# Filter network of a long convolution: chunk by chunk instead of four chunks at a time, with its decay moved into two tables

## What is computed

```python
h_mlp  = np.maximum(pos_emb @ w1, 0.0) @ w2          # 12480 x 64 -> 64 -> 128
window = np.exp(-0.01 * pos)[:, None]
h_filt = h_mlp * window
u  = x * v                                            # 12480 x 128
Uf = np.fft.rfft(u, n=L, axis=1)                      # L = 2 * 12480
Hf = np.fft.rfft(h_filt, n=L, axis=0)
y  = np.fft.irfft(Uf * Hf[None, :, :], n=L, axis=1)[:, :S, :]
x1 = x * y
x2 = np.maximum(x1 @ moe_w_in, 0.0) ** 2 @ moe_w_out  # 128 -> 2048 -> 128
h  = x2 @ moe2_w_in
out = (h / (1 + np.exp(-1.702 * h))) @ moe2_w_out
```

## Time and profile before

| | us |
|---|---|
| median of 3 runs (lowest, highest) | 1559.16 (1558.95, 1559.96) |
| the profiled execution's own time | 1559.6 |
| its span, first to last instruction | 1557.8 |
| start of the first transform in it | 62.73 |
| TensorE busy in the span | 1532.8 |
| VectorE, ScalarE, GpSimd busy | 992.7, 943.0, 270.0 |
| mean granted TensorE clock | 0.998 of full speed |

### The profile page before, as it was taken

The page is one execution under the profiler, slowest core; times in us unless marked ns, Lnnn a source line. Parts: engine busy times, 40 slices in busy tenths (PEclk is TensorE's granted clock), DMA queues, the critical chain, the costliest instruction groups (busy, mean ns, idle before and its releaser), DMA issues.

```text
span 1557.8 us, 22645 instructions
## 1 busy us (share of the span) xinstructions
PE 1532.8 (98%) x7860; PEld 1458.2 (94%) x7860; DVE 992.7 (64%) x1315; ACT 943.0 (61%) x1217; POOL 270.0 (17%) x313
## 2 busy tenths in 40 slices
PE   7999999999989999999999999999999999999998
PEld 5898889988779999999999999999999999999997
DVE  4867686676656666666666666666666666666664
ACT  3353003431067777777777777777777777777775
POOL 5706791177710000000000000000000000000000
PEclk9999999999999999999999999999999999999999
DMA  7454720743000000000000000000000000000000
GB/s 179 110 83 126 138 41 26 115 113 105 1 0 1 7 10 5 5 5 5 5 5 5 5 5 5 5 5 5 5 5 5 5 5 6 10 5 5 5 7 11
DMA packets 93769, 46.89 MB, mean 30 GB/s; under 512 B 77705, under 2 KB 89337, under 8 KB 93481
## 3 DMA queue, kind: packets, MB, share of 16 engines
q1 hardware_dynamic: 92670, 45.80, 13.2%
q10 hardware_dynamic: 1067, 0.66, 0.1%
HBM read 40.06 MB, written 6.39 MB: 30 GB/s over the span
## 4 chain that ended last, share of the span: by engine, by line
PE 95%; DVE 3%; ACT 1%; issue 1%; DMA 0%; SPq 0%; ACTq 0%; DVEq 0%
PE ps L965 23%; PE ps L967 23%; PE ps L966 23%; PE ps L685 7%; PE ps L737 7%; PE ps L718 6%; PE ps L746 3%; DVE big L561 1%; PE ps L959 1%; PE ps L659 1%; PE ps L673 1%; PE ps L953 1%; PE ps L664 1%; DVE act_lo L940 0%; ACT act_f L890 0%
## 5 line engine op out<-in xcount | busy, mean ns | idle before, releaser
L940 DVE TENSOR_TENSOR act_lo<-act_f,act_hi 128x832 fp32r<-128x832 f32 x480 | 487.0, 1025 | 129.8 <-ACT act_hi L895 121.6
L965 PE MATMUL ps<-act_hi,w_hi 128*128 128x416 f32 x960 | 344.0, 358 | 1.3 <-DVE act_lo L940 1.3
L965 PE MATMUL ps<-in_hi,w_hi 128*128 128x416 f32 x960 | 337.8, 352 | 5.7 <-DVE in_lo L911 3.9
L967 PE MATMUL ps<-act_hi,w_lo 128*128 128x416 f32 x960 | 338.3, 352 | 0.0
L966 PE MATMUL ps<-in_lo,w_hi 128*128 128x416 f32 x960 | 336.0, 350 | 0.0
L966 PE MATMUL ps<-act_lo,w_hi 128*128 128x416 f32 x960 | 335.5, 349 | 0.0
L967 PE MATMUL ps<-in_hi,w_lo 128*128 128x416 f32 x960 | 334.1, 348 | 0.0
L938 DVE CAST act_hi<-act_f 128x832 fp32r<-128x832 f32 x240 | 148.4, 618 | 288.4 <-ACT act_f L890 288.4
L885 ACT ACTIVATE relu<-ps 128x832 f32<-128x832 f32 x240 | 208.3, 868 | 142.7 <-PE ps L967 138.8
L892 ACT ACTIVATE act_f<-ps 128x832 f32<-128x832 f32 x240 | 207.0, 863 | 117.7 <-PE ps L967 117.6
L890 ACT ACTIVATE act_f<-relu 128x832 f32<-128x832 f32 x240 | 216.0, 900 | 22.2 <-DVE act_lo L940 0.3
(11 more groups left out here) (64 smaller groups left out, 1401.2 us busy)
## 6 DMA issues: line engine op xcount, KB each, us to landing
f_ring<-in_fwd SPq DMA_DIRECT2D x52, 240.0 KB, 2.6
u_buf<-in_x SPq DMA_DIRECT2D x20, 312.0 KB
big<-in_v SPq DMA_DIRECT2D x20, 312.0 KB
filter_then_xy<-in_x SPq DMA_DIRECT2D x8, 780.0 KB
out<-rows SPq DMA_DIRECT2D x30, 208.0 KB
big<-in_pos_emb SPq DMA_DIRECT2D x40, 78.0 KB
u_buf<-in_moe_w_in SPq DMA_DIRECT2D x2, 1024.0 KB, 7.5
t<-in_inv ACTq DMA_DIRECT2D x1, 168.8 KB
```

What stands on the lines that cost most here:

```text
L940: nc.vector.tensor_tensor(lo[:, :, :], f[:, :, :], hi[:, :, :].bitcast(F32), ALU.subtract)\
L965: nc.tensor.matmul(to, w_hi[w][:, cols], hi, start=first, stop=False)
L967: return nc.tensor.matmul(to, w_lo[w][:, cols], hi, start=False, stop=last)
```

## The change

- `window` is gone. Since exp(-0.01(120a + b)) is a product of a factor in a and one in b, the factor in b (positive) becomes the per-partition `scale` of the rectification, which is now three ScalarE instructions of 104 columns per chunk (one per pair of positions), and the factor in a goes into a second version of the first transform's table, used for the filter. `t1` holds both and has its own place in SBUF.
- With no window to multiply, `taps` is gone. ScalarE copies the upper three positions of a chunk to SBUF (`copy_high`, 104x384), and VectorE forms both the sum and the difference from PSUM and that copy; GpSimd's part in the network is gone.
- The loops over rounds are written out chunk by chunk on all engines: TensorE does the transposes of chunk n+2, the first layer of n+1 and the second layer of n.
- All of `pos_emb` has a place in SBUF, so its loads wait for nothing. Ten chunks are loaded ahead of the first piece of u, then five chunks and a piece in turn.
- w1, w2 in block-diagonal form and the scales come as one transfer of 128x444; the other tables are loaded from ScalarE's queue behind chunk 4. VectorE folds pieces 0, 1, 2 behind chunks 9, 14, 19, and pieces 3, 4 at groups 3 and 7 of the first transform.
- Four spare products instead of twelve stand ahead of the first transform.

```diff
-    window = np.exp(np.float32(-0.01) * np.arange(S, dtype=np.float32)).reshape(A, B)[:, order]
+    decay_b = np.exp(-0.01 * b)[order].reshape(NCH * HB, 2).T
+    decay_a = np.exp(-0.01 * B * a)
+    net = np.concatenate([twice(w1), twice(w2), np.repeat(decay_b, FO, axis=0)], axis=1)
+    return {"fwd1": np.concatenate([fwd1, fwd1 * decay_a[:, None]], axis=1), "fwd2": fwd2, "inv3": inv3,
...
     @block.sync
-        for i in range(ROUNDS):
-            for s in range(RING):
-                load_pe(i, s)
-            if i > 0:
-                load_x_piece(0, i - 1)
-                load_v_piece(0, i - 1)
-        load_x_piece(0, PIECES - 1)
-        load_v_piece(0, PIECES - 1)
+        PE_AHEAD = 2 * PIECES
+        for n in range(NCH):
+            load_pe(n)
+            if n + 1 >= PE_AHEAD and (n + 1) % PIECES == 0:
+                i = (n + 1 - PE_AHEAD) // PIECES
+                load_x_piece(0, i)
+                load_v_piece(0, i)
+        for i in range(3, PIECES):
+            load_x_piece(0, i)
+            load_v_piece(0, i)
...
     @block.gpsimd
-                pool.wait_ge(free[s], i + 1)
-                nc.gpsimd.tensor_tensor(h_rows(BR - (n + 1) * HB, BR - n * HB), by_half(taps[:, s, 0:HB])[:, ::-1],
-                                        by_half(taps[:, s, HB:CB]), ALU.subtract).then_inc(h_odd[s], 1)
-            if i > 0:
-                make_u(0, i - 1)
-        make_u(0, PIECES - 1)
+        for i in range(PIECES):
+            make_u(0, i)
...
     @block.scalar
+            for j in range(HB):
+                cols = slice(j * A, (j + 1) * A)
+                last = nc.scalar.activation(hid[:, s, cols], slot[s][:, 1, cols], ACT.Relu, scale=decay[:, n, j:j + 1])
+            last.then_inc(hid_relu[s], 1)
...
+            nc.scalar.copy(high_rows[:, s].rearrange("p b h c -> p (b h c)"), flat[s][0:A, HB * D:CB * D])\
+                .then_inc(high_copied[s], 1)
...
+        for n in range(NCH):
+            if n + 2 < NCH:
+                copy_pe(n + 2)
+            if n + 1 < NCH:
+                relu_hid(n + 1)
+            copy_high(n)
+            if n == RING:
+                act.dma_start(t1[:, :, :].rearrange("p k w -> p (k w)"), fwd1).then_inc(tables_in, 16)
...
     @block.vector
-                nc.vector.tensor_tensor(
-                    taps[:, s], flat[s][0:A, 0:CB * D].rearrange("p (b c) -> p b c", b=CB),
-                    win[:, n * CB:(n + 1) * CB].unsqueeze(2).to_broadcast([A, CB, D]), ALU.mult).then_inc(free[s], 1)
-                dve.wait_ge(free[s], i + 1)
-                nc.vector.tensor_tensor(h_rows(n * HB, (n + 1) * HB), by_half(taps[:, s, 0:HB]),
-                                        by_half(taps[:, s, HB:CB])[:, ::-1], ALU.add).then_inc(h_even[s], 1)
+        FOLD_BEHIND = {9: 0, 14: 1, 19: 2}
...
+            dve.wait_ge(high_copied[s], i + 1)
+            nc.vector.tensor_tensor(h_rows(n * HB, (n + 1) * HB), low, high[:, ::-1], ALU.add)
+            nc.vector.tensor_tensor(h_rows(BR - (n + 1) * HB, BR - n * HB), low[:, ::-1], high, ALU.subtract)\
+                .then_inc(free[s], 1)
+            if n in FOLD_BEHIND:
+                fold_u(0, FOLD_BEHIND[n])
...
     @block.tensor
-                mm = nc.tensor.matmul(slot[q][0:BR, e // 2, at:at + 2 * A], data, t1[:, :],
+                mm = nc.tensor.matmul(slot[q][0:BR, e // 2, at:at + 2 * A], data, t1[:, 1 if k < N1 // 2 else 0, :],
...
-        filter_network(0)
-        with pe.Fori(1, ROUNDS) as i:
-            filter_network(i)
+        transpose_pe(0)
+        transpose_pe(1)
+        pe.wait_ge(net_in, 16 * NET_LOADS)
+        first_layer(0)
+        for n in range(NCH):
+            if n + 2 < NCH:
+                transpose_pe(n + 2)
+            if n + 1 < NCH:
+                first_layer(n + 1)
+            second_layer(n)
...
-                for s in range(RING):
+                for s, spare in enumerate((1, 1, 2, 0)):
                     pe.wait_ge(free[s], used["s1", 0][s])
-                    spare_products(s, 3)
-                for s in range(RING):
-                    pe.wait_ge(h_even[s], ROUNDS)
-                    pe.wait_ge(h_odd[s], ROUNDS)
+                    spare_products(s, spare)
```

More of the change, by code:

```diff
@@ L153, in convolution @@
 def convolution(nc, block, sem, ALU, ACT, ds, F32, H, ps, u_buf, buf, weights, first_tile,
-                x_d, v_d, pe_d, w1, w2, fwd1, fwd2_d, inv3, twiddle, inv4, window, identity):
+                x_d, v_d, pe_d, net, fwd1, fwd2_d, inv3, twiddle, inv4, identity):
     first_in, stage, mlp_ident, mlp_ident_in, staged, in_trans = first_tile
@@ L476, in _ @@
     def _(act):
-        def filter_copies(i):
-            for s in range(RING):
[L479 to L487, removed]
@@ L499, in _, with copy_pe, relu_hid @@
[L499 to L502, removed]
+        def copy_pe(n):
+            s, i = n % RING, n // RING
+            act.wait_ge(pe_trans[s], i + 1)
+            after(act, hid_made[s], i)
+            nc.scalar.copy(peT[:, s], slot[s][:, 0, 0:HB * A]).then_inc(pe_copied[s], 1)
+        def relu_hid(n):
+            s, i = n % RING, n // RING
+            act.wait_ge(hid_made[s], i + 1)
+            after(act, full[s], i)
+            for j in range(HB):
+                cols = slice(j * A, (j + 1) * A)
+                last = nc.scalar.activation(hid[:, s, cols], slot[s][:, 1, cols], ACT.Relu, scale=decay[:, n, j:j + 1])
+            last.then_inc(hid_relu[s], 1)
@@ new lines, in copy_high @@
+        def copy_high(n):
+            s, i = n % RING, n // RING
+            act.wait_ge(full[s], i + 1)
+            after(act, free[s], i)
+            nc.scalar.copy(high_rows[:, s].rearrange("p b h c -> p (b h c)"), flat[s][0:A, HB * D:CB * D])\
+                .then_inc(high_copied[s], 1)
+        act.dma_start(ident, identity).then_inc(ident_in, 16)
+        act.dma_start(big[0:128, w_at:net_at], net).then_inc(net_in, 16)
+        copy_pe(0)
+        copy_pe(1)
+        act.wait_ge(net_in, 16 * NET_LOADS)
@@ L644, in _ @@
         pe.wait_ge(ident_in, 16)
[L645 to L660, removed]
-            for s in range(RING):
-                pe.wait_ge(hid_relu[s], i + 1)
-                for j in range(HB):
-                    mm = nc.tensor.matmul(flat[s][0:A, j * 2 * D:(j + 1) * 2 * D], hid[:, s, j * A:(j + 1) * A],
-                                          w2bd.rearrange("p e n -> p (e n)"), start=True, stop=True)
-                mm.then_inc(full[s], 1)
@@ new lines, in transpose_pe, with first_layer @@
+        def transpose_pe(n):
+            s, i = n % RING, n // RING
+            pe.wait_ge(ld_pe[n], 2 * 16)
+            after(pe, free[s], i)
+            for j in range(HB):
+                mm = nc.tensor.transpose(slot[s][0:128, 0, j * A:(j + 1) * A],
+                                         pe_rows[:, n, 2 * j:2 * j + 2, :].rearrange("p b c -> p (b c)"),
+                                         ident[0:A, 0:A])
+            mm.then_inc(pe_trans[s], 1)
+        def first_layer(n):
+            s, i = n % RING, n // RING
+            pe.wait_ge(pe_copied[s], i + 1)
+            nc.tensor.matmul(slot[s][:, 1, 0:HB * A], w1bd.rearrange("p e n -> p (e n)"), peT[:, s],
+                             start=True, stop=True).then_inc(hid_made[s], 1)
@@ L668, in _, with second_layer @@
+        def second_layer(n):
+            s, i = n % RING, n // RING
+            pe.wait_ge(hid_relu[s], i + 1)
+            for j in range(HB):
+                mm = nc.tensor.matmul(flat[s][0:A, j * 2 * D:(j + 1) * 2 * D], hid[:, s, j * A:(j + 1) * A],
+                                      w2bd.rearrange("p e n -> p (e n)"), start=True, stop=True)
+            mm.then_inc(full[s], 1)
         t4_row = t4[:, :, :].rearrange("p r a -> p (r a)")
@@ L1033 @@
     arrays, args = {}, []
-    given = [(n, inputs[n]) for n in _INS] + [(n, t.astype(np.float32)) for n, t in constant_tables().items()]
+    given = [(n, inputs[n]) for n in _INS] + [(n, t.astype(np.float32)) for n, t in constant_tables(inputs["w1"], inputs["w2"]).items()]
     for name, a in given:
```

80 lines of the change are left out of this document (33 added, 47 removed).

## The result

The changed kernel takes **1555.37 us** (median of 10 runs, 1552.03 to 1556.28) against 1559.37 for the kernel before (10 runs), a ratio of 0.9971, 95% interval 0.9963 to 0.9979. By the medians that is 4.0 us or 0.26% faster (0.29% by the ratio): in the direction that was forecast and inside the range of 1548.2 to 1557.2, but 3.2 us short of the predicted 1552.2.

A forecast was written before the change was run, and what follows sets the result against it. TensorE was taken to bound the kernel, busy 1532.8 of 1557.8 us. Terms 5.6 + 43.2 + 2.1 + 3.0 + 1.8 put the first transform at 55.7 against 62.73, 7.0 earlier: 1552.2 us, range 1548.2 to 1557.2.

The forecast's parts named there:

- the forecast's own case: Whole kernel: the first transform starts 7.0 us earlier, giving 1552.2; a gain of 4 to 9, chance 0.60.
- 1 start of the first layer: Head of the network: the first layer waits for two chunks and net; 5.6 us, between 4.9 and 7.5.
- 2 TensorE's work: Network on TensorE: 20 chunks of 2.19 less 0.64 for two sets of transposes done before; 43.2 us.
- 3 cold clock: Head of the network: TensorE starts at 1.2 GHz before reaching 2.4; 2.1 us lost, between 1 and 4.
- 4 per-chunk waits: Each chunk: slot free 1.8 us behind its full and ScalarE's 1.7, both inside 2.19; cost 0.
- 5 first fold: Behind chunk 9: fold meets GpSimd making piece 1, takes 4.2 and stalls chunk 14's transposes 2.6 us.
- 5 second fold: At about 45 us, as GpSimd ends piece 2 and ahead of piece 3: short fold, stall 0.2 us.
- 5 tables: Four table transfers issued by ScalarE in iteration 4: 1.6 us in a slack of about 1.5; 0.2 added.
- 6 tail: Behind the last second layer: slot free 1.8 us later, hiding four spare products; 1.8 against some 4.1 before.
- ScalarE as the bound: Rival, network loop: slow scaled rectifications make a chunk 2.7 us instead of 2.19; 1562.2 us, chance 0.04.
- term 5: Folds and table transfers in the network loop: 3.0 us together, between 0.4 and 7.2.
- part of a rival: Rival, network loop: two long folds, and TensorE's clock falls after each stall; gain 1.2, 1558.0 us, chance 0.14.

The follow-up runs named there:

- the loads' order: The changed kernel with the loads queued in the order of before, four chunks and a piece in turn, without the waits: 1551.83 us.
- the three together: The changed kernel with folds behind chunks 7 and 12, table transfers one by one, and products of zeroed rows ahead of the network: 1548.36 us.
- the kernel in fours: The changed kernel with TensorE and ScalarE going through the network four chunks at a time, step by step as before: 1557.16 us.

## Why the prediction was right, and where it was off

The time fell into the range, but not by the forecast's mechanism alone. The prediction named as a sign of being wrong that "the granted clock falls in the loop", and it did. It also expected the idle time ahead of chunk 14 and next to none at chunk 19; there were 1.78 and 2.27. Its gain of 4.0 is the very edge of the forecast's own case (4 to 9). By its terms, in us:

| term | forecast | measured |
|---|---|---|
| 1 start of the first layer | 5.6 | 5.76 |
| 2 TensorE's work | 43.2 | 41.6 (20 x 2.11 less 0.56) |
| 3 cold clock | 2.1 | 2.0 (10.43 - 5.76 = 4.67, later 2.66) |
| 4 per-chunk waits | 0 | 0 |
| 5 first fold | 2.6 | 1.8 |
| 5 second fold | 0.2 | 2.3 |
| 5 tables | 0.2 | 0.8 |
| clock in the loop | 0 | 1.6 |
| 6 tail | 1.8 | 1.6 |
| sum | 55.7 | 57.5; start at 58.20 |

Of the 0.7 that no row holds, 0.5 is this: from one chunk's transposes to the next the two waits cost 1.94 and 2.44, not 1.78 and 2.27, and the tail from the first spare product to the transform is 1.79. Part of the result is luck: TensorE's work and the first fold came out 1.6 and 0.8 below the forecast and hid as much of what the second fold, the tables and the clock cost more.

- **Right**: that TensorE becomes the bound and no chunk waits; VectorE's pair takes 0.555 and 0.547 in the mean (forecast 0.56), the pair ends 1.6 behind the second layer (forecast 1.8); ScalarE is well below the period. Its scaled rectification of 104 columns shows as 0.348 (mean), three in a row as 0.82, so 0.24 apart; with 0.27 each I had the three at 0.81. ScalarE as the bound is out.
- **Right**: that the stretch behind passes the shift on, and that the spare products held the old tail to its end (GpSimd was done 1.1 us before them).
- **The step that failed** is term 5, "ahead of piece 3: the short one, 0.2". Piece 2 was ready for GpSimd at 43.27, not at 41, as the transfers moved at less than 200 GB/s (184 and 181 in the stretches from 8 and 27); the fold came at 44.46, in its midst. The tables, which land between, were also larger than I reckoned: `t1` holds two versions, so the four are 0.53 MB and not 0.44, about 0.45 us at 200 GB/s. The two kernels in which the folds no longer meet GpSimd's pieces, or barely (folds at 7 and 12; the loads' order) gain 4.7 and 3.5 us of median. They shorten the first wait too (1.78 to 0.16 and 0.38), so the second meeting's own share is read from the rows: 2.1 of waiting and the 1.6 of the clock behind it, more than the 3.2 of the miss. The first fold's 2.6 was too much for the same reason: piece 1 landed late, and the fold's first half was through before it.
- The clock's fall was in the text as part of a rival only. It took 1.6 us, half of the miss. In the text I tied it to the pauses of rounds in fours, "here it is a single one"; here a single pause of 2.27 stood before the fall.
- The tables: ScalarE was 1.76 late, near my 1.6, but TensorE lost 0.83, so the slack was 0.9 and not 1.5. The slack I had was TensorE's; ScalarE's own order put a copy behind the transfers that the next chunk but one needed.
- **Arithmetic of the recorded text**: a chunk of 2.19 was formed from the lengths of merged rows, which hold the end of the last product (0.97 / 3 and 5.34 / 4). From start to start the second layers are 36.80 - 31.62 = 5.18 apart, 1.295 each, and in the changed kernel three transposes take 0.28 (14.65 to 14.93), which gives the measured 2.11. And term 5's upper bound of 7.2 does not follow from its parts: twice 2.6 and 4 x 1.80 less 1.5 are 10.9.
- The rule on the shared ports (Trainium skill, SBUF — State Buffer, "Who interferes with whom") agrees with the rows here: in the changed kernel GpSimd's first operation ran from 32.58 for 1.8 (half of an undisturbed 3.58) to 34.4, and L555, issued at 32.80, ended at 32.80 + 2.57 = 35.37, which is 34.4 and a whole 0.95. My estimate by its worst phase, a fold of 5.4, did not occur; the longest took 5.0 (57.91 to 62.91 with the three together). The pair with an operand in PSUM was not held in any profiled execution (0.54 to 0.56 throughout, also beside GpSimd at 28.75 to 31.9 in the run with the loads' order).

## What to carry to other kernels

When two engines exclude each other, place one's long operations in the gaps of the other's, by the trace and not by the sum of busy times: here neither engine was full, and moving two folds by two chunks was worth 4.7 us, more than the 4.0 that the rewrite had brought with them in the wrong place. Executions that scatter in groups can point to such a race between a transfer's landing and an instruction; here the scatter went when the meetings did (1.05 us instead of 5.4). Count an issue of transfers on a compute engine's queue against the next thing that this engine owes, not against the slack of the engine that waits.

## What the runs showed of the hardware

- At the start products take double time with the clock column at 1.00 (1.08 against 0.55 for a first layer), while a fall later on shows there (0.60 over 50 to 54 us).
- With four products on zeroed rows ahead the full pace came 1.2 us earlier (mean of three executions against six).
- Pauses of 2.2 to 2.3 us at 47 to 50 us were followed by a fall in the changed kernel and with twelve spare products, but not in the kernel in fours (2.21 before 49.71), and 1.78 before 46.05 not with the products ahead. The kernel before had two shorter pauses, 0.86 and 1.00 between 46.9 and 49.2, and 0.57 over 50 to 54 behind them; 1.81 before 65.13 with the three together was followed by 0.50. So the length of a pause alone does not decide it; what does stays open.
